# Attention's chunk edges: half sums added between two k-tiles, the second half of v loaded in two parts, ranks and scatters moved one step earlier

## What is computed

```python
scores = (1.0 / S) * np.matmul(z, z.transpose(0, 2, 1))
attn = np.maximum(scores, 0.0) ** 2
x = (u * np.matmul(attn, v)).reshape(B * S, D)
# layer 1: only rows with x @ w_skip > 0; the others stay x
e = argmax(x @ w_gate);  x += gate * (relu(x @ w1[e]) @ w2[e])
# layer 2: all rows, a bias per modality on the logits
e = argmax(x @ w_gate2 + bias[modality]);  out = gate * (relu(x @ w1_2[e]) @ w2_2[e])
```

## Time and profile before

| what | value |
|---|---|
| median of 3 runs | 1529.11 us (1528.56 to 1531.15) |
| profiled execution, its own time | 1530.26 us |
| span of its profile | 1528.5 us, 34462 instructions |
| attention (first chunk to last sums) | about 0 to 726 us |
| mean granted TensorE clock | 0.991 |
| HBM traffic | 107 MB, mean 70 GB/s |

### The profile page before, as it was taken

How to read it: one execution, slowest core, us unless ns; L and a number is a source line. 1 busy time by engine, 2 the same in 40 slices (tenths; PEclk the granted TensorE clock), 3 DMA queues, 4 the chain that set the end, 5 groups by cost and what they waited for, 6 DMA issues and landing times.

```text
span 1528.5 us, 34462 instructions
## 1 busy us (share of the span) xinstructions
PE 1484.9 (97%) x11777; PEld 1290.2 (84%) x11777; DVE 1010.1 (66%) x2375; ACT 770.9 (50%) x1504; POOL 396.0 (26%) x370
## 2 busy tenths in 40 slices
PE   8999999999999999999899999998999999999995
PEld 7778878788878888788799999997888888888884
DVE  7989977899779988977666666673333333333332
ACT  6676766676667767665344444442332333333331
POOL 4133322334223424212222222221511211211211
PEclk9999999999999999999999999999999999999998
DMA  5311030212212020200533353322211111111110
GB/s 118 97 32 62 28 98 28 64 40 56 84 32 64 28 84 27 85 30 31 168 107 134 134 179 129 103 94 69 97 49 49 42 64 48 42 46 53 42 46 24
DMA packets 57743, 107.27 MB, mean 70 GB/s; under 512 B 17863, under 2 KB 32210, under 8 KB 57612
## 3 DMA queue, kind: packets, MB, share of 16 engines
q0 software_dynamic: 18192, 58.13, 11.0%
q1 hardware_dynamic: 39420, 47.48, 10.8%
HBM read 75.63 MB, written 31.49 MB: 70 GB/s over the span
## 4 chain that ended last, share of the span: by engine, by line
PE 83%; DVE 5%; issue 4%; DMA 3%; ACT 2%; POOL 1%; SPq 0%; POOLq 0%; DVEq 0%; ACTq 0%
PE pO L1359 25%; PE pS L1625 11%; PE pO L1637 10%; PE pS L1563 9%; PE pO L1546 9%; PE pS L1348 7%; PE pO L1639 5%; PE pM L1625 4%; DVE AH L1031 3%; DMA raw<-in_v_dram 2%; PE pT L1600 1%; DMA token_rows<-xrow,dest 1%; PE pT L1407 1%; DVE AL L1033 1%; PE pT L1495 1%
## 5 line engine op out<-in xcount | busy, mean ns | idle before, releaser
L1033 DVE TENSOR_TENSOR AL<-A,AH 128x512 fp32r<-128x512 f32 (+1 forms) x400 | 307.1, 768 | 13.7
L1359 PE MATMUL pO<-AH,VH 64*128 64x512 f32 (+1 forms) x1520 | 298.9, 384 | 8.0 <-DVE xT L941 6.1
L1359 PE MATMUL pO<-AH,VL 64*128 64x512 f32 (+1 forms) x1520 | 297.5, 382 | 0.0
L1359 PE MATMUL pO<-AL,VH 64*128 64x512 f32 (+1 forms) x1520 | 297.3, 382 | 0.0
L672 ACT ACTIVATE R<-pS 128x512 f32<-128x512 f32 (+1 forms) x400 | 213.3, 587 | 157.3 <-PE pS L1348 140.1
L1031 DVE CAST AH<-A 128x512 fp32r<-128x512 f32 (+1 forms) x400 | 233.8, 584 | 43.1 <-ACT A L681 42.3
L681 ACT ACTIVATE A<-R 128x512 f32<-128x512 f32 (+1 forms) x400 | 229.2, 624 | 17.7 <-DVE AL L1033 17.5
L1637 PE MATMUL pO<-VL,AH 128*128 128x512 f32 x640 | 232.4, 399 | 0.0
L1298 DVE SCALAR_TENSOR_TENSOR AL<-pS,AH 128x512 fp32r<-128x512 f32 x120 | 82.9, 692 | 186.0 <-ACT AH L862 185.3
L1639 PE MATMUL pO<-VL,AL 128*128 128x256 f32 x640 | 179.4, 280 | 0.0
L1359 PEld LDWEIGHTS pO<-AH,VH 64*128 64x128 f32 x1520 | 147.2, 184 | 35.3 <-issue 10.8
(11 more groups left out here) (218 smaller groups left out, 2416.1 us busy)
## 6 DMA issues: line engine op xcount, KB each, us to landing
raw<-in_w_dram POOLq DMA_DIRECT2D x22, 1024.0 KB
A<-token_rows SPq DMA_DIRECT2D x21, 536.0 KB, 3.6
uT<-in_u_dram SPq DMA_DIRECT2D x16, 512.0 KB
A<-in_w2t_dram POOLq DMA_DIRECT2D x8, 1024.0 KB
xin<-token_rows SPq DMA_DIRECT2D x24, 268.0 KB
raw<-in_v_dram SPq DMA_DIRECT2D x4, 1152.0 KB, 5.8
raw<-in_v_dram SPq DMA_DIRECT2D x4, 768.0 KB, 7.9
raw<-in_z_dram SPq DMA_DIRECT2D x8, 368.0 KB
```

The costliest lines, as they stand in the source:

```text
L1033: v_.tensor_tensor(AL[k % NBUF][:, 0:n], A[k % NA][:, 0:n], AH[k % NBUF][:, 0:n].bitcast(F32), ALU.subtract).then_inc(al_ready, 1)
L1359: last = t_.matmul(pO[:, (KD * r + d) * QW:(KD * r + d) * QW + n], vv[rows, vo + k * D + d * P:vo + k * D + (d + 1) * P], a[k % NBUF][rows ...
```

## The change

Five things change in the attention, and one in the second expert phase:

1. The second half of v is loaded in two parts, k-tiles 10 to 13 once two `v_low` pieces are done, and 14 to 19 once five are (for all four batches), with a semaphore of its own for the first part.
2. ACT makes pieces 5 to 9 of VH after steps 5, 6, 7, 8, 9 of chunk c=3, no longer after steps 1, 3, 5, 7, 9.
3. DVE adds the half accumulators between the splits of k-tiles 2 and 3 of the new chunk, one split earlier than before.
4. `place_rows(g-1)` moves from after step 2 to after step 0 on DVE, the second `xrow_half` from after step 1 to after step 0 on ACT, and on POOL `scatter_chunk(g-1)` now stands ahead of `times_u(g)`.
5. PE's `route_rows` and `prefixes` move from after step 7 to after step 6.
6. In the second expert phase ACT makes the next expert's high parts also where an expert has no tile (an `Else` branch).

```diff
@@ -192,6 +192,7 @@
         v_first_loaded = [sem(f"v_first_loaded{i}") for i in range(2)]
         z_loaded = [sem(f"z_loaded{i}") for i in range(len(Z_PARTS))]
         v_loaded = sem("v_loaded")
+        v_mid_loaded = sem("v_mid_loaded")
         u_loaded = sem("u_loaded")
         zh_ready = sem("zh_ready")
         zl_ready = sem("zl_ready")
@@ -310,7 +311,8 @@
                     vb = v[b, :, :]
                     full, at = min(k1, KT - 1), k0 % VHALF
                     to = vraw[:, at * D:(at + full - k0) * D].rearrange("p (j d) -> p j d", d=D)
-                    sp.dma_start(to, vb[k0 * P:full * P, :].rearrange("(j p) d -> p j d", p=P)).then_inc(v_loaded if k0 >= FIRST else v_first_loaded[k0 * 2 // FIRST], 16)
+                    sp.dma_start(to, vb[k0 * P:full * P, :].rearrange("(j p) d -> p j d", p=P)).then_inc(
+                        v_first_loaded[k0 * 2 // FIRST] if k0 < FIRST else v_mid_loaded if k0 == VHALF else v_loaded, 16)
                     if k1 == KT:
                         for r in range(2):
                             sp.dma_start(vraw[r * H:(r + 1) * H, (VHALF - 1) * D:VHALF * D], vb[full * P:S, :]).then_inc(v_loaded, 16)
@@ -321,8 +323,10 @@
                 load_v(0, FIRST // 2, FIRST)
                 load_z(0, 2)
                 load_v(0, FIRST, VHALF)
+                sp.wait_ge(vl_ready, 2)
+                load_v(0, VHALF, VHALF + 4)
                 sp.wait_ge(vl_ready, VU // 2)
-                load_v(0, VHALF, KT)
+                load_v(0, VHALF + 4, KT)
                 sp.wait_ge(zeroed, 1)
                 sp.dma_start(wg[:, :, 0:E], w_gate.rearrange("(k p) e -> p k e", p=P)).then_inc(consts_loaded, 16)
                 sp.dma_start(wg[:, :, E:E + 1], w_skip.rearrange("(k p o) -> p k o", p=P, o=1)).then_inc(consts_loaded, 16)
@@ -356,8 +360,10 @@
                             load_v(b + 1, FIRST // 2, FIRST)
                             load_v(b + 1, FIRST, VHALF)
                         if c == 2 and b < B - 1:
+                            sp.wait_ge(vl_ready, VU * b + VU + 2)
+                            load_v(b + 1, VHALF, VHALF + 4)
                             sp.wait_ge(vl_ready, VU * b + VU + VU // 2)
-                            load_v(b + 1, VHALF, KT)
+                            load_v(b + 1, VHALF + 4, KT)
 
                 for ph in range(2):
                     q = PH[ph]
@@ -536,10 +542,10 @@
                 v_low(0, n)
             for g in range(CHUNKS):
                 b, c = divmod(g, QC)
+                if g > 1:
+                    scatter_chunk(g - 1)
                 if g > 0:
                     times_u(g)
-                if g > 1:
-                    scatter_chunk(g - 1)
                 if g == (B - 1) * QC:
                     wait(zl_ready, NG * B)
                     load_weights(0)
@@ -659,7 +665,10 @@
                 if 2 * n < FIRST:
                     act.wait_ge(v_first_loaded[n], 16 * b + 16)
                 else:
-                    act.wait_ge(v_loaded, 64 * b + (16 if 2 * n < VHALF else 64))
+                    if VHALF <= 2 * n < VHALF + 4:
+                        act.wait_ge(v_mid_loaded, 16 * b + 16)
+                    else:
+                        act.wait_ge(v_loaded, 64 * b + (16 if 2 * n < VHALF else 64))
                 s_.copy(VH[:, to:to + 2 * D], vraw[:, at:at + 2 * D]).then_inc(vh_ready, 1)
 
             def relus(g, p, n):
@@ -703,17 +712,17 @@
                             if p == 1:
                                 act.wait_ge(pv_done, KT * QC * b + NBUF)
                             v_high(b + 1, p // 2)
-                        elif c == QC - 2:
-                            v_high(b + 1, VU // 2 + p // 2)
                         elif c == QC - 1:
                             z_high(b + 1, p // 2)
+                    if p >= VU // 2 and b < B - 1 and c == QC - 2:
+                        v_high(b + 1, p)
                     if g == (B - 1) * QC + 1 and p % 2 == 1 and p // 2 < WP:
                         if p == 1:
                             act.wait_ge(pv_done, KT * QC * (B - 1) + NBUF)
                         split_high(0, 0, p // 2)
                     if p == 6 and g > 0:
                         xrow_half(g, 0)
-                    if p == 1 and g > 1:
+                    if p == 0 and g > 1:
                         xrow_half(g - 1, 1)
             xrow_half(CHUNKS - 1, 1)
             def copy_gcols(e):
@@ -878,6 +887,10 @@
                                         split_high(turn_ + 1, 1 - h, n)
                             for s in range(SUB2):
                                 low_part(t, t % 2, s)
+                    with act.Else():
+                        with act.If(hi < total):
+                            for n in range(WP):
+                                split_high(turn_ + 1, 1 - h, n)
                     lo = hi
                 act.wait_ge(q.stored, STORED + 16 * SUB2 * total)
                 act.sem_inc(act_passed, 1)
@@ -1019,13 +1032,18 @@
                 if 2 * n < FIRST:
                     dve.wait_ge(v_first_loaded[n], 16)
                 else:
-                    dve.wait_ge(v_loaded, 16 if 2 * n < VHALF else 64)
+                    if VHALF <= 2 * n < VHALF + 4:
+                        dve.wait_ge(v_mid_loaded, 16)
+                    else:
+                        dve.wait_ge(v_loaded, 16 if 2 * n < VHALF else 64)
                 v_.tensor_copy(VH[:, w], vraw[:, at:at + 2 * D]).then_inc(vh_ready, 1)
 
             def split(g, p, n):
 
                 for k in (2 * p, 2 * p + 1):
                     at = KT * g + k
+                    if k == 2 * AHEAD - 3 and g > 0:
+                        add_sums(g)
                     dve.wait_ge(square_done, at + 1)
                     dve.wait_ge(pv_done, at + 1)
                     v_.tensor_copy(AH[k % NBUF][:, 0:n], A[k % NA][:, 0:n]).then_inc(ah_ready, 1)
@@ -1051,14 +1069,12 @@
                             token_table()
                         if g == 1 and p in (3, 4, 5):
                             bias_table(p - 3)
-                        if p == AHEAD - 2:
-                            add_sums(g)
                         if p == 7:
                             pick_experts(g)
                         if p == 8:
                             row_meta(g)
                             set_gates(g)
-                        if p == 2 and g > 1:
+                        if p == 0 and g > 1:
                             place_rows(g - 1)
                         if p == 9 and g == CHUNKS - 1:
                             place_rows(g)
@@ -1461,7 +1477,7 @@
                     if g > 0:
                         if p == 3:
                             route(g)
-                        if p == 7:
+                        if p == 6:
                             route_rows(g)
                             prefixes(g)
```

## The result

The changed kernel takes **1533.7 us** (median of 7 runs, 1530.75 to 1535.81); the kernel before took 1529.2 us (7 runs, 1528.32 to 1531.15). The ratio is 1.0028, 95% interval 1.0018 to 1.0039: slower by 4.5 us. The forecast was 1525.2 us, faster, with a range that ended at 1531.5. Sign and range were both missed; the third rival, a cast held behind POOL's row at the edges, described what happened.

The account below looks back on a forecast made before the run. PE, busy 97% of the span, was taken as the bound, its attention waits costing 14.7 us at most. Gains of −7.6 and costs of +3.7 gave −3.9 us, so 1525.2 us against the median; range 1518.5 to 1531.5.

Parts of the forecast that it names:

- the third rival: The slower rival: cast of k-tile 3 or 5 held behind POOL's row at every edge; about 1535 us, chance 0.13.
- start: Chunk 0: with k-tiles 10 to 13 loaded earlier, DVE reaches VH's piece 5 sooner and PE resumes as much sooner; −0.6 us.
- edge of chunk 1: Additions come one split sooner, with no ranks placed there, shortening PE's wait of 1.26 us; −1.1 us.
- loads, chunks 3, 8, 13: Edges of these chunks: nothing on ACT waits any longer for the second half of v; −3.1 us.
- chunks 5, 10, 15 (landing, additions): Scatters land sooner for ACT's copy at 5 and 10, −1.4 us; earlier additions nearly cancelled by ranks at three edges, −0.4.
- edge of chunk 17: POOL's first weight subtractions follow the splits one by one and don't pile up behind the scatters; −1.0 us.
- `prefixes`, chunk 16: One step earlier, PE waits 2 us for the one-hot matrix, but the wait only changes its place; 0.
- order: chunks 6, 11: Cast of k-tile 3 is held behind a scatter and `times_u`, delaying PE 0.8 us at each; +1.6 us.
- order: chunks 2, 7, 12: The first product starts before the second addition ends, so the cast gets in; 0.2 us each.
- order: chunks 4, 9, 14: Two products and two z subtractions (5.0 us) may hold k-tile 5 for 2 us; +1.0 us for the three.
- DVE's turn between POOL's instructions: Rival: DVE gets in between POOL's instructions, so the +3.7 us vanish; 1518.8 to 1523 us, chance 0.25.
- PE's waits for the one-hot matrix outside chunk 16: Rival: the edges' waits go to `prefixes`, 5.4 us lost in chunks 3 and 4 of three batches; about 1529, chance 0.15.

Follow-up runs that it names:

- order back: Changed kernel with POOL's `times_u(g)` ahead of `scatter_chunk(g-1)` again, all else kept; 1518.42 us, ratio 0.9929 against the kernel before.
- the ranks back: Changed kernel with POOL's old order, and ranks (after step 2) and second copy of rows (after step 1) as before; 1526.38 us, ratio 0.9989.
- the spaced kernel: Changed kernel, scatters still ahead, but each `times_u` product and the first low parts behind it wait for a split of the chunk; 1518.94 us, ratio 0.9935.
- the products alone: Changed kernel with only the first low parts of v and z made to wait, so the two `times_u` products still follow each other; 1525.77 us, ratio 0.9984.

## Why the prediction was wrong

The terms against the table above, in us; where the prediction gave one term for several chunks, so does this. The last column is the kernel "order back":

| term | predicted | changed kernel | order back |
|---|---|---|---|
| start | −0.6 | −0.7 | −0.6 |
| edge of chunk 1 | −1.1 | −1.1 | −1.1 |
| loads, chunks 3, 8, 13 | −3.1 | −2.9 | −4.3 |
| chunks 5, 10, 15 (landing, additions) | −1.8 | −4.7 | −4.2 |
| edge of chunk 17 | −1.0 | −0.7 | −0.7 |
| `prefixes`, chunk 16 | 0 | +0.2 | −0.2 |
| order: chunks 6, 11 | +1.6 | +0.7 | 0 |
| order: chunks 2, 7, 12 | +0.6 | **+6.5** | 0 |
| order: chunks 4, 9, 14 | +1.0 | **+6.4** | 0 |
| order: chunks 18 and 19 | +0.5 | +1.7 | 0 |
| attention's end | −3.9 | +5.4 | −11.0 |

**What held.** The start and the edge of chunk 1 came out as counted: PE's wait of 1.21 us in the earlier trace rows became 0.52, and the additions' longest wait (1.26 us) became 0.19. The waits of the earlier trace rows fell away. That the loads gave the 3.1 us predicted (2.9) was luck: by themselves they give 4.2, and the changed kernel lost 1.4 of it again in chunks 3 and 13. Chunk 6 was right in its mechanism: predicted were scatters from about 225.7 us, `times_u` at 230.8 and a hold to 233.3; there are 226.24, 231.32 and a hold of 3.40 us to 234.43. Its price was 0.4 us and not 0.8.

**The step that failed first** is this one: "At chunks 2, 7 and 12 the first product starts before the second addition ends, so the cast gets in; 0.2 us each". It is wrong twice. *The timing:* in the changed kernel the first product starts 0.75 us after the second addition ended (86.20 against 85.45), not 0.3 us before it: the scatters come about 1 us later than I counted. The kernel with `prefixes` after step 7 starts them at 80.24 instead of 81.13 us with the additions at the same times (82.72, 84.76): PE's transposes and prefixes of the finished chunk now stand ahead of the scores that the next chunk's first splits, ranks and scatters hang on. I counted that move only as a wait for the one-hot matrix. *The rule:* in that kernel the product starts before the addition ends, by 0.28 us in chunk 2 and 0.48 in chunk 7, and the cast is held for 3.88 and 3.70 us. The earlier trace rows were read as "the second addition was not finished"; what they show is a POOL that had come from a wait for DVE. A term of 0.6 us was 6.5.

**The second** is "a row of two products and two z subtractions (5.0 us) may hold k-tile 5 for 2 us ... I take half of the rest and of the doubt". The row came, it held a split for up to 6.02 us, and PE waited 1.85 us in chunk 4, 0.3 + 0.2 in chunk 9 and 1.90 in chunk 14. What the prediction hoped to get back at the following edges did come back, and more (−4.7 for −1.8), but "order back" gets the same 4.2 us there without the row. It was thus no credit of the hold, and should have stood among the gains. The landing of the earlier trace rows goes when ranks and scatters come sooner: with both put back it costs PE 1.3 us at each of chunks 5 and 10. DVE's lag of the earlier trace rows, 0.8 to 0.9 us of wait at each of the three edges, is 0.4 to 0.5 with the new loads alone, under 0.2 with the ranks sooner as well, and gone with the additions' new place, with or without the ranks.

**The third** is what the prediction said would be held: the cast. The subtraction of a split is held as well (4.70 us at 85.82), so it didn't help that the cast of k-tile 3 was through before the row began.

**The rivals.** The slower rival named the mechanism and the point of decision (a mean of 0.42 us over 18 edges). By the chunk times it cost 16.5 us against "order back" (729.42 less 712.94), 0.9 us an edge; its 13.8 was near, its sum of +6 too, since it was set against gains of 7.6 where there were 11. It was given 0.13 because "the timing in chunks 2, 7, 12 favours the cast by 0.3 us": a margin smaller than the error of the count. DVE's turn between POOL's instructions did not happen in any row that followed scatters. PE's waits for the one-hot matrix outside chunk 16 appeared only in experiments: with the ranks back (0.53 us in chunks 4 and 9), in the spaced kernel (0.3 us in chunks 4, 9 and 14), and with the products alone (0.16 us in chunk 4).

**The signs.** ACT's waits for v were gone, and DVE instructions of over 2.5 us stood behind the edges of chunks 3 (3.56), 6 (3.40) and 8 (3.06). PE's row for relus did not fall (4.0 us), the expected 2 us wait at the ranks of chunk 16 wasn't there, and of the sign "if PE waits for AL in steps 1 and 2 in most chunks" the waits showed a part: there are seven, in chunks 2, 4, 7, 9, 12, 14 and 19, the largest in 4 and 14. Few edges carried the loss.

## What to carry to other kernels

When a reordering lets an engine find its elementwise instructions all ready, price the whole row as one instruction against a neighbour that it was seen to hold, and put the row where that neighbour has lead. The worst place in these runs was right behind the point where PE changes its input. Waits on the neighbour's own progress between the instructions were as good as the old order within the noise (1518.94 us against 1518.42). And when a step is moved, redo the timing of everything that hangs on the engine that it moved on: a term that rests on a margin of 0.3 us is not known, and its other end belongs in the middle of the forecast.

## What the runs showed of the hardware

- **A held instruction waits for the whole row.** Four rows of 2, 3, 4 and 5 POOL instructions of about 1.25 us each held one DVE instruction for 3.48, 4.70, 5.89 and 6.90 us. The Trainium skill, page "SBUF — State Buffer", section "Who interferes with whom", has the shared port pair held for one whole instruction; none of the rows behind scatters goes by that, though a single product does (1.66 us for a subtraction of 0.69 beside it).
- **Not only casts.** Subtractions with both inputs in SBUF are held in the same way (4.70 and 6.02 us in the changed kernel). The additions read PSUM: in the kernel before, one ran its usual 0.69 us from 86.50 beside a product from 85.81 to 87.10.
- **A long wait can cost twice.** In the attention, behind waits of PE of 2.18, 2.23 and 2.65 us the granted clock fell to 0.51 to 0.56 for 3 to 4 us; behind one of 2.19 us it did not. What decides it stays open.
- **The same offset, two outcomes.** At the edge of chunk 1 in "order back" POOL came from a wait for DVE, and the second addition ended 0.48 us after the first product began: the two products took 2.73 us and the cast 1.17. In chunk 7 of the kernel with `prefixes` back, POOL came from a scatter, the offset was the same 0.48 us, the products took 2.56 us and the cast 3.70. In the traces of these kernels every pair of products behind a wait for the additions let DVE in, and every unspaced pair behind scatters did not. What POOL does differently stays open.
